# A decayed attention and two feed-forward layers on one core: the seventh Strassen-type product ahead of the second, and a new order of loads and VectorE work in the attention

## The reference, cut to what matters

```
for each block of 64 rows:                        # 2 batches, 8 heads, 768 rows, width 64
    intra = ((q k^T) * Dmask) v                   # Dmask[i,j] = lam^(i-j) for i >= j
    inter = (q * lam^(pos+1)) state
    out   = intra + inter
    state = lam^64 * state + (k * lam^(63-pos))^T v
x = out as [1536, 512]
p = probs / (sum(probs) + 1e-9)
x = sum over 4 experts e of  p[:, e] * (relu(x @ w1[e]) @ w2[e])     # w1 512x1024, w2 1024x512
h = x @ w_in;  out = (h * cos(h)) @ w_out                           # 512x2048, 2048x512
```

## Time and profile before

| | us |
|---|---|
| median of 3 runs | 815.4 (815.35 to 815.62) |
| the profiled execution | 815.58 |
| its span, first to last instruction | 813.8 |
| PE busy in it | 802.8 |
| attention, to the first matmul of the expert layer | 0 to 48.88 |
| steps 0 and 1 of the expert layer | 48.88 to 78.64 |

### The profile page before, as it was taken

One profiled execution on the slowest core, in us unless ns is written; L12 is line 12 of the kernel. 1 busy time (PEld: TensorE's weight loads), 2 busy tenths in 40 slices (PEclk: granted clock), 3 DMA queues, 4 the chain that ended last, 5 costly groups with the idle time before them and its releaser, 6 DMA issues.

```text
span 813.8 us, 11375 instructions
## 1 busy us (share of the span) xinstructions
PE 802.8 (99%) x4404; PEld 677.9 (83%) x4404; DVE 584.4 (72%) x964; ACT 292.0 (36%) x548; POOL 225.7 (28%) x228
## 2 busy tenths in 40 slices
PE   8989999999999999999999999999999999999998
PEld 7878888888888888888888888888888888888886
DVE  6988767767667657657667667677777777777766
ACT  4743222322322322322322222246545454555442
POOL 4955433433433433433433433242000000000000
PEclk9999999999999999999999999999999999999999
DMA  9941211111101121011111011001011011100004
GB/s 325 334 136 40 65 28 39 39 66 39 40 27 39 27 78 39 27 39 40 27 39 39 26 40 39 27 27 26 27 39 39 27 27 39 38 27 27 1 0 155
DMA packets 19865, 44.83 MB, mean 55 GB/s; under 512 B 2344, under 2 KB 2392, under 8 KB 19812
## 3 DMA queue, kind: packets, MB, share of 16 engines
q1 hardware_dynamic: 19812, 44.10, 17.0%
HBM read 40.93 MB, written 3.17 MB: 54 GB/s over the span
## 4 chain that ended last, share of the span: by engine, by line
PE 96%; DMA 2%; DVE 1%; POOL 0%; issue 0%; ACT 0%; SPq 0%; DVEq 0%
PE ps L982 32%; PE ps L963 28%; PE ps L1043 16%; PE ps L1062 16%; DMA att<-att_in 2%; PE ps L880 1%; PE ps L930 1%; PE ps L904 1%; PE ps L917 1%; PE ps L894 1%; DVE w_lo L673 0%; DVE temps L729 0%; POOL h_lo L422 0%; DVE att L633 0%; DVE temps L724 0%
## 5 line engine op out<-in xcount | busy, mean ns | idle before, releaser
L422 POOL TENSOR_TENSOR h_lo<-temps,h_hi 128x512 fp32r<-128x512 f32 (+1 forms) x128 | 135.1, 1056 | 298.7 <-ACT h_hi L518 298.7
L518 ACT ACTIVATE h_hi<-temps 128x512 fp32r<-128x512 f32 (+1 forms) x128 | 67.3, 525 | 338.9 <-DVE temps L729 338.9
L712 DVE TENSOR_TENSOR y<-ps,y 128x512 f32<-128x512 f32 x180 | 124.1, 689 | 71.7 <-PE ps L982 71.7
L963 PE MATMUL ps<-x_hi,w_hi 128*128 128x512 f32 (+1 forms) x448 | 150.4, 336 | 2.5 <-DVE temps L762 2.2
L982 PE MATMUL ps<-h_hi,w_hi 128*128 128x512 f32 x384 | 150.5, 392 | 0.8 <-POOL h_lo L422 0.8
L963 PE MATMUL ps<-x_hi,w_lo 128*128 128x512 f32 (+1 forms) x448 | 150.5, 336 | 0.0
L963 PE MATMUL ps<-x_lo,w_hi 128*128 128x512 f32 (+1 forms) x448 | 150.5, 336 | 0.0
L982 PE MATMUL ps<-h_lo,w_hi 128*128 128x512 f32 x384 | 150.4, 392 | 0.0
L982 PE MATMUL ps<-h_hi,w_lo 128*128 128x512 f32 x384 | 149.4, 389 | 0.0
L963 PEld LDWEIGHTS ps<-x_hi,w_hi 128*128 128x128 f32 x448 | 84.7, 189 | 15.2 <-DVE temps L762 2.6
L963 PEld LDWEIGHTS ps<-x_lo,w_hi 128*128 128x128 f32 x448 | 84.7, 189 | 11.7
(11 more groups left out here) (83 smaller groups left out, 1115.9 us busy)
## 6 DMA issues: line engine op xcount, KB each, us to landing
w_raw<-w_in SPq DMA_DIRECT2D x96, 256.0 KB, 2.6
att<-att_in SPq DMA_DIRECT2D x24, 512.0 KB, 6.4
temps<-p_scr SPq DMA_DIRECT2D x4, 768.0 KB, 4.0
out<-y SPq DMA_DIRECT2D x12, 256.0 KB, 2.0
att<-dp_in SPq DMA_DIRECT2D x1, 24.0 KB
p_scr<-att SPq DMA_DIRECT2D x1, 24.0 KB
lam<-lam_in SPq DMA_DIRECT2D x1, 6.0 KB, 1.8
```

Source lines behind the costliest of these rows:

```text
L422: pool.tensor_tensor(hs_lo[side][:, f, at], ring(s, i), f32(hs_hi[side][:, f, at]), ALU.subtract).then_inc(s_hlo, 1)
L518: act.activation(hs_hi[s % SIDES][:, f, at], ring(s, i), ACT.Copy).then_inc(s_hhi, 1)
L712: dve.tensor_tensor(at, from_bank, at, ALU.add).then_inc(s_y, 1)
L963: mm = pe.matmul(ps[:, bank, 0:CTS[side]], ww[q % 2][:, of], xx[side][:, 2 * x + k, :], start=(opens and k == 0 and n == 0), stop=(k == 1 ...
```

## The change

- The product order is P1, P6, P5, P7, P2, P4, P3 in all 32 steps. In side 0, down 0 now follows P5 and down 1 follows P7, and none follows P2; in side 1, down 0 follows P5, down 1 P7, downs 2 and 3 P2. Step 1 has its own list (`FOLLOW_FIRST`): 0 and 1 after P2, 2 to 4 after P4, 5 to 7 after P3. DVE's order follows: v2, v3, sum_of 1, a down piece, weighted 0.
- The first weights of the second product (w2 of quarter 0) are split during the attention: high parts by ACT and low parts by POOL in block 4, where DVE made the low parts in step 0.
- `qk(0)` is loaded in two halves of 256 KB; `scores(0)` starts on the first. After `kv(0)` come now `qk(2)`, `kv(1)`, `dps` (before: `dps`, `kv(1)`, `qk(2)`).
- DVE: the four scans for `qpow` are put around mask(1); in each block `k_decay(2p+3)` goes behind both masks; `x_parts` becomes `x_sums` (four sums) and `x_lows` (two low parts); the last piece of the first w1 weights goes between x_sums(4) and x_lows(4); x_lows(5) goes behind v2 of step 0. ACT does t_high(4) before x_high(5).
- PE's wait for the low parts of the x combinations (`s_tlo`) moves from P1 to P6.

```diff
-P1, P6, P5, P2, P7, P4, P3 = range(7)
+P1, P6, P5, P7, P2, P4, P3 = range(7)
-FOLLOW = (((), (), (), (0,), (1,), (2,), (3,)), ((), (), (0,), (1,), (2, 3), (4, 5), (6, 7)))
+FOLLOW = (((), (), (0,), (1,), (), (2,), (3,)), ((), (), (0,), (1,), (2, 3), (4, 5), (6, 7)))
+FOLLOW_FIRST = ((), (), (), (), (0, 1), (2, 3, 4), (5, 6, 7))
...
+            def load_qk0(half, signal):
+                at = slice(D // 2 * half, D // 2 * (half + 1))
+                sp.dma_start(qk[:, 0, :, at], att_in[0, :, 0:2, at]).then_inc(signal, 16)
...
-            load_qk(0)
+            load_qk0(0, s_qk_half)
+            load_qk0(1, s_qk[0])
             load_qk(1)
             load_kv(0)
+            load_qk(2)
+            load_kv(1)
             sp.dma_start(dps, dp_in).then_inc(s_dp, 16)
-            load_kv(1)
-            load_qk(2)
...
+            def w2_low(i):
+                hi, lo, raw = w2_split(0, i)
+                pool.wait_ge(s_whi, w2_count(0, i))
+                pool.wait_ge(s_wlo, w1_count(0) + i)
+                pool.tensor_tensor(lo, raw, f32(hi), ALU.subtract).then_inc(s_wlo, 1)
...
+                if p == BLOCKS - 2:
+                    w2_low(0)
+                    w2_low(1)
...
+                if p:
+                    t_high(p - 1)
                 if 0 < p < BLOCKS - 1:
-                    t_high(p - 1)
                     new_state(p)
                 x_high(p)
...
+                if p == BLOCKS - 2:
+                    w2_piece(0, 0)
+                    w2_piece(0, 1)
...
             for p in range(1, BLOCKS):
-                x_parts(p - 1)
+                x_sums(p - 1)
+                if p == BLOCKS - 1:
+                    w1_piece(0, 2)
+                x_lows(p - 1)
+                if p + 1 < BLOCKS:
+                    mask(2 * p + 2)
+                    if p == 1:
+                        dve.wait_ge(s_norm, 1)
+                        dve.reciprocal(dsum[:, :], dsum[:, :]).then_inc(s_norm, 1)
+                    if 2 <= p <= 3:
+                        w1_piece(0, p - 2)
+                    mask(2 * p + 3)
                 if p + 2 < BLOCKS:
                     k_decay(2 * p + 3)
...
-                dve.wait_ge(s_prod, 7 * s + P2 + 1)
+                dve.wait_ge(s_prod, 7 * s + P7 + 1)
+                dve.tensor_tensor(v3, bank_b, p1, ALU.add).then_inc(s_u, 1)
...
+                sum_of(s, 1, bank_c, v3)
+                if s == 1:
+                    down(0, 0)
                 if side == 1:
                     down(s - 1, 1)
                 else:
                     down(s - 1, 0)
-                dve.wait_ge(s_prod, 7 * s + P7 + 1)
-                dve.tensor_tensor(v3, bank_b, p1, ALU.add).then_inc(s_u, 1)
-                dve.wait_ge(s_u, 2 * s + 2)
-                sum_of(s, 1, bank_c, v3)
+                dve.wait_ge(s_prod, 7 * s + P2 + 1)
+                weighted(s, 0, bank_a)
...
-                    if i == P5 and side == 1:
+                    if i == (P2 if s == 1 else P5) and side == 1:
                         pe.wait_ge(s_wlo, w2_count(q, 1))
```

More of the change, by code:

```diff
@@ L37 @@
 STEPS = SIDES * QUARTERS
-P1, P6, P5, P2, P7, P4, P3 = range(7)
-PRODUCTS = ((0, 0, 0, True), (4, 4, 1, True), (3, 3, 2, True), (1, 1, 0, False), (5, 5, 1, False),
+P1, P6, P5, P7, P2, P4, P3 = range(7)
+PRODUCTS = ((0, 0, 0, True), (4, 4, 1, True), (3, 3, 2, True), (5, 5, 1, False), (1, 1, 0, False),
             (2, 6, 1, False), (6, 2, 2, False))
-FOLLOW = (((), (), (), (0,), (1,), (2,), (3,)), ((), (), (0,), (1,), (2, 3), (4, 5), (6, 7)))
+FOLLOW = (((), (), (0,), (1,), (), (2,), (3,)), ((), (), (0,), (1,), (2, 3), (4, 5), (6, 7)))
+FOLLOW_FIRST = ((), (), (), (), (0, 1), (2, 3, 4), (5, 6, 7))
 DOWNS = (8, 4)
@@ L154, in build @@
         s_qk = [sem(f"s_qk{i}") for i in range(QK)]
+        s_qk_half = sem("s_qk_half")
         s_kv = [sem(f"s_kv{i}") for i in range(KV)]
@@ L530, in _ @@
                 if s == 0:
-                    t_high(BLOCKS - 2)
                     t_high(BLOCKS - 1)
-                    w2_piece(0, 0)
                     h_high(s, 0)
-                    w2_piece(0, 1)
                     h_high(s, 1)
@@ L645, in k_decay, with x_sums @@
                                   ALU.mult).then_inc(s_kd[1], 1)
-            def x_parts(p):
-                side, at = x_columns(2 * p)
+            def x_sums(p):
                 b0, b1 = x_of(2 * p), x_of(2 * p + 1)
@@ L657, in x_parts, with x_lows @@
                 dve.tensor_tensor(t2, b1[:, 1, :, :], t1, ALU.subtract).then_inc(s_tsum, 1)
+                dve.wait_ge(s_tsum, 4 * p + 3)
+                dve.tensor_tensor(t4, b0[:, 1, :, :], t2, ALU.subtract).then_inc(s_tsum, 1)
+            def x_lows(p):
+                side, at = x_columns(2 * p)
+                b0, b1 = x_of(2 * p), x_of(2 * p + 1)
                 dve.tensor_tensor(tiles(xs_lo[side][:, 0:4, at]), b0, f32(tiles(xs_hi[side][:, 0:4, at])),
                                   ALU.subtract).then_inc(s_xlo, 1)
-                dve.wait_ge(s_tsum, 4 * p + 3)
-                dve.tensor_tensor(t4, b0[:, 1, :, :], t2, ALU.subtract).then_inc(s_tsum, 1)
                 dve.tensor_tensor(xs_lo[side][:, 4:6, at], b1[:, 1, :, :], f32(xs_hi[side][:, 4:6, at]),
@@ L673, in w2_piece, with q_powers @@
                 dve.tensor_tensor(lo, raw, f32(hi), ALU.subtract).then_inc(s_wlo, 1)
[L675 to L678, removed]
+            def q_powers(a):
                 dve.tensor_tensor_scan(qpow[:, a, :], lam[:, HEADS + a:HEADS + a + 1].to_broadcast([P, P]),
                                        zeros, 1.0, ALU.mult, ALU.add).then_inc(s_tab, 1)
+            mask(0)
+            q_powers(0)
+            q_powers(1)
+            mask(1)
+            q_powers(2)
+            q_powers(3)
+            k_decay(1)
             mask(2)
             mask(3)
-            dve.wait_ge(s_norm, 1)
-            dve.reciprocal(dsum[:, :], dsum[:, :]).then_inc(s_norm, 1)
             k_decay(3)
             for p in range(1, BLOCKS):
-                x_parts(p - 1)
+                x_sums(p - 1)
[10 more added lines that the diff above has]
+                    mask(2 * p + 3)
                 if p + 2 < BLOCKS:
                     k_decay(2 * p + 3)
[L690 to L698, removed]
+            x_sums(BLOCKS - 1)
             def down(s, i):
@@ L741, in _ @@
                 dve.tensor_tensor(v2, bank_b, p1, ALU.add).then_inc(s_u, 1)
+                if s == 0:
+                    x_lows(BLOCKS - 1)
                 if s == 1:
@@ L748, in _ @@
                     w2_piece(q + 1, 0)
-                if side == 1:
+                if side == 1 and s > 1:
                     down(s - 1, 0)
-                dve.wait_ge(s_prod, 7 * s + P2 + 1)
+                dve.wait_ge(s_prod, 7 * s + P7 + 1)
+                dve.tensor_tensor(v3, bank_b, p1, ALU.add).then_inc(s_u, 1)
                 if 4 * s >= R_RING:
                     dve.wait_ge(s_hlo, 4 * s - R_RING + 1)
-                weighted(s, 0, bank_a)
-                if s == 0:
-                    w2_piece(0, 0)
+                dve.wait_ge(s_u, 2 * s + 2)
+                sum_of(s, 1, bank_c, v3)
+                if s == 1:
+                    down(0, 0)
                 if side == 1:
@@ L872, in scores @@
                 s = n % QK
-                pe.wait_ge(s_qk[s], 16 * (n // QK + 1))
-                if n >= 1:
+                if n == 0:
+                    pe.wait_ge(s_qk_half, 16)
+                else:
+                    pe.wait_ge(s_qk[s], 16 * (n // QK + 1))
                     pe.wait_ge(s_mask, 2 * n - 1)
                 for a in range(PAIRS):
+                    if n == 0 and a == PAIRS // 2:
+                        pe.wait_ge(s_qk[0], 16)
                     for par in range(2):
@@ L996, in _ @@
                             pe.wait_ge(s_xlo, 2 * sum(SIDE_BLOCKS[:side + 1]))
-                            pe.wait_ge(s_tlo, sum(SIDE_BLOCKS[:side + 1]))
                         if s >= 1:
@@ L1001, in _ @@
                         pe.wait_ge(s_wlo, w1_count(0))
+                    if i == P6 and q == 0:
+                        pe.wait_ge(s_tlo, sum(SIDE_BLOCKS[:side + 1]))
                     if i == P6 and s >= 1:
                         pe.wait_ge(s_t, 3 * s - 1)
-                    if i == P5 and side == 1:
+                    if i == (P2 if s == 1 else P5) and side == 1:
                         pe.wait_ge(s_wlo, w2_count(q, 1))
@@ L1017, in _ @@
                     product(s, i)
-                    for d in FOLLOW[side][i]:
+                    for d in (FOLLOW_FIRST if s == 1 else FOLLOW[side])[i]:
                         down(s - 1, d)
```

## The result

The changed kernel takes 828.6 us (median of 4 runs, 826.6 to 829.6) against 815.4 us before (815.1 to 815.6): ratio 1.0159, 95% interval 1.0139 to 1.0179. It is slower, as forecast, but by 13.2 us where 6.7 were forecast, and above the end of the range at 825.0. The profiled execution took 826.59 us, with a span of 824.8 us. Its span is 11.0 us longer than that of before.

What follows compares the result with a forecast made beforehand. PE, busy 99% of the span, was taken as the bound. Attention -0.65, steps 0 and 1 -1.95 and steady steps +9.3 summed to +6.7 us, 822.1 us; own range 818.5 to 825, 8-in-10 range 812.3 to 825.

Steps and rivals of the forecast that it cites:

- The steady steps: Steps 2 to 31: each of 15 side-1 steps loses 0.62 us (bounds 0 and 0.9), +9.3 us in all.
- Steps 1 to 3 of its chain: Steady steps: DVE's row just fits, h_low 0 moves to 306.66 into w1 piece 1, and DVE and POOL take turns.
- step 4: Steady steps, turns applied: w1 piece 1 ends at 308.55, weighted 2 at 310.25, weighted 3 at 313.1 instead of about 312.17.
- The sign that I had named: Changed profile's list of PE waits: P7 waits for v2 about 15 times, 0.3 to 0.9 us each.
- the opening step: Whole kernel: PE is busy 99% of the span, so any new wait of PE is lost one for one.
- rival (c): Attention and steps 0 and 1: late w2 low parts and late dps eat both gains; 824.7 us, chance 0.07.
- The mask: Attention: mask(4) no longer stands behind k_decay(5), so scores(5) follows from_scores(3) at once; -1.09 us, bounds 0 and 1.1.
- The dps term: Attention: dps lands about 11.4 instead of 8.89, delaying the q_decays and scores(4); +0.45 us, bounds 0 and +0.8.
- Steps 0 and 1: First two expert steps: P4's 2.18 us wait goes, P7 of step 1 is next; -1.95 us, between -1.2 and -2.8.
- (a): Rival: w1 piece 1 slips in before h_low 0, no steady loss; 812.8 us, 811.5 to 814.2, chance 0.25.
- (b): Rival: waits of 0.1 to 0.25 us in 15 steps cancel the start's gain; 814.3 to 817 us, chance 0.13.
- The rows at 79 us: Kernel before's trace: POOL's sum ran between two queued DVE weight pieces, taken to show a second DVE instruction doesn't exclude POOL.

Runs made afterwards that it cites:

- masks_only: The kernel before with one edit, the key decay behind both masks in each attention block: 814.53 us, ratio 0.9988.
- dps_back: The changed kernel with the old product order from step 2 on and the dps load right behind kv(0) again: 813.56 us, ratio 0.9976.
- after_again: The changed kernel run once more, unedited, for its median: 827.38 us (4 runs), ratio 1.0145.
- prod1_first: The changed kernel with ACT taking prod1 of the side-1 step before h_high 3 of the step before: 822.43 us (1 run).
- low01_cleared: The changed kernel with h_low 0 and 1 of side-0 steps from 2 on replaced by memsets: 814.57 us (1 run).
- both_fixes: The changed kernel with w1 piece 1 right behind piece 0 and prod1 taken before h_high 3: 816.88 us (11 runs), 1.0019 of before.
- low0_cleared: The changed kernel with only h_low 0 of side-0 steps from 2 on replaced by a memset: 824.98 us (1 run).
- new_on_before: The kernel before with the new product order and DVE's new order in steps 2 to 31 alone: 827.81 us, ratio 1.0148.
- piece1_early: The changed kernel with w1 piece 1 made right behind piece 0, out of POOL's way: 823.67 us (1 run).

## Why the prediction was wrong in size

**The steady steps: right mechanism, the term was mis-sized.** "The side-1 step loses 0.62 us" measured 0.83. Steps 1 to 3 of its chain held within 0.01 us: h_low 0 starts at 306.65 in the prediction's times (306.66 forecast) and w1 piece 1 ends at 308.55, as forecast. Then step 4 failed by its own adding up. sum 2 starts at 308.47, as forecast, and at 0.60 us apiece weighted 2 starts at 309.67 and ends 0.68 later at 310.35, where I wrote 310.25; the trace has 310.35 (218.59 + 0.68). sum 3 then ends at 312.09 and weighted 3 at 313.29, where I wrote 313.1. That makes 0.19 us, most of the missing 0.21, with no new behaviour behind it; the rest is small change between the end of v2 and the start of P7. The 0.1 for a restarted PE was right (0.11). The sign that I had named, 15 waits of 0.3 to 0.9 us, came as 15 waits of 0.19 us on average, and the opening step, that a wait of PE is lost one for one, was wrong: idle time of 5.3 us stands against a loss of 12.5. 15 x 0.21 = 3.2 us, half of what the whole forecast lacks.

**The range.** The upper bounds of the three terms were +13.5 (0.9 per step), 0 and -1.2; their sum, +12.3, ends at 827.7. I closed the range at 825.0, with rival (c), and so left the bound of the largest term out. Even 827.7 is 0.9 below the median.

**The start: one half right, one half too cheap.** The mask was worth what was forecast: from scores(4) to scores(5) are 4.14 us in after (18.78 to 22.92) against 5.30 before, and masks_only alone gave -1.1 us. The dps term was +0.45 forecast. The timeline of after, POOL:

```profile
12.11 0.76 POOL L375 TENSOR_TENSOR dsum<-att 12x128 f32<-12x128 f32 x1 [10.64 <-DMA att<-dp_in]
...
14.61 2.50 POOL L363 TENSOR_TENSOR att<-att 128x512 f32<-128x512 f32 x2
```

and PE:

```profile
17.16 0.67 PE L927 MATMUL ps<-att 64*64 64x128 f32 x16 [0.57 <-POOL att L363]
...
18.78 1.16 PE L913 MATMUL ps<-att 64*128 64x128 f32 x16
...
26.43 1.16 PE L913 MATMUL ps<-att 64*128 64x128 f32 x16 [0.29 <-DMA att<-att_in]
```

dps landed at 12.1, not 11.4, and everything behind it followed as computed: scores(4) at 18.78 (18.15 forecast, 17.70 before), +1.08. That is past the bound that I had named for a slipped landing (+0.8): it slipped by 0.7 us, not by a third. Then came a cost that I had not seen, since of the late q_decay I followed only PE's wait: SP waits for it too, because qk(5) goes into the buffer of qk(2). SP's issues in after:

```profile
9.23 0.51 SPq L294 DMA_DIRECT2D att<-att_in  x1
15.97 0.33 SPq L287 DMA_DIRECT2D att<-att_in  x1
16.39 0.38 SPq L294 DMA_DIRECT2D att<-att_in  x1
16.82 0.90 SPq L304 DMA_DIRECT2D w_raw<-w_in  x2
17.82 0.92 SPq L287 DMA_DIRECT2D att<-att_in  x1
```

qk(5) is issued at 15.97 (13.93 before), right behind the end of q_decay(2) at 15.88, and the queue behind it goes late: kv(5), two weight pieces, and qk(6) at 17.82 (16.90 before). qk(6) lands 8.57 us later, at 26.39, and scores(6) waits 0.29 us. 0.63 and 0.29 turn -0.65 into about +0.3, which is the measured +0.30. dps_back gives about 1 us back: its q_decay(2) starts at 11.50, and it issues qk(5) at 12.86.

**Steps 0 and 1: right.** -1.79 measured, -1.95 forecast, with the collisions where they were put: the timeline of DVE in after, 57 to 62 us, has weighted 1 (L758) stretched by POOL's last t_low, which ends at 57.83, and weighted 2 and 3 by its h_lows. They end 0.5 to 0.6 us later than forecast, 0.3 of it from the later start. P7 of step 1 then waits 1.51 us for v2:

```profile
57.12 1.27 DVE L758 SCALAR_TENSOR_TENSOR temps<-temps 128x512 f32<-128x512 f32 x1
...
59.02 1.07 DVE L758 SCALAR_TENSOR_TENSOR temps<-temps 128x512 f32<-128x512 f32 x1
...
60.73 1.06 DVE L758 SCALAR_TENSOR_TENSOR temps<-temps 128x512 f32<-128x512 f32 x1
```

**The sum.** Forecast +6.7; the profiled execution has +0.3 - 1.8 + 12.5 = +11.0. The terms miss by 1.0, 0.2 and 3.2. The median lies 2.0 us above the profiled execution, while after_again's lies 0.5 above its own. The three slower runs of the first four (828.2 to 829.6 us) have a mean granted clock of 0.997 to 0.998; the fastest and all four of after_again (826.6 to 827.5) have 1.000. A mean of 0.998 over 825 us is one stretch of 3.3 us at half clock, an estimate, and such a stretch cost prod1_first 1.56 us (last section). That fits most of the 2.0, but these three runs have no trace, so it is not shown. Of the rivals, (a) and (b) are refuted by the 15 waits; (c) is refuted as a whole, since steps 0 and 1 kept their gain, but its half about the late dps was true.

**The rule of the Trainium skill.** That a VectorE instruction with two SBUF inputs and a GpSimd instruction that reads SBUF exclude each other was what gave the forecast its sign (the Trainium skill, "SBUF — State Buffer", "Who interferes with whom"). The traces agree: 0.42 to 1.53 us, and back to 0.41 in low01_cleared. The rows at 79 us, two DVE instructions in a row and POOL between them, carried over to the side-0 steps, where h_low 0 gets in ahead of w1 piece 1. They are no law, though: in the attention of both_fixes a DVE instruction lost its turn (below).

## What to carry to other kernels

Before moving a matmul forward, follow its operand back through the in-order queues: here P7's v2 hung on prod1, which stood behind h_high 3 on ACT, and P2 and down 1 had hidden that. A row of DVE work that just fits has no room for a single collision with POOL, and taking away one collision may only hand the time to the next; count a wait from start to start of PE's work, not by the idle time that the list shows: the list had 5.3 of 12.5 us, and none of the last 0.12 per quarter. A small load on which a queue of POOL work waits should not be put behind large ones, above all where later loads wait for that work to free their buffers.

## What the hardware showed that was not expected

- A POOL memset, which reads no SBUF, beside DVE work with two SBUF inputs costs the DVE work nothing: it runs beside a weighted of 0.68 and a weight piece of 0.42, and it takes 0.52 to 0.53 us itself in all 45 cases of low0_cleared and low01_cleared.
- DVE and POOL do not always take turns. In both_fixes, `k_decay(5)` (L667) waited while two POOL instructions ran one after the other, and took 2.90 us where it took 1.44 in after:

```profile
25.60 2.90 DVE L667 TENSOR_TENSOR att<-att,kpow 128x512 f32<-128x512 f32 x1
...
25.46 1.26 POOL L384 TENSOR_TENSOR att<-att,dsum 12x512 f32<-12x512 f32 x1
26.69 1.26 POOL L363 TENSOR_TENSOR att<-att 128x512 f32<-128x512 f32 x1
```

  prod1_first shows the same (2.66 us). In masks_only and low0_cleared the same pair met the same DVE instruction without a pause either, and DVE got its turn between them (1.81 and 1.43 us). In after a pause of 0.24 us lay between the two, since the second one's load landed late, and DVE went first. What decides the turn is open.
- After a pause of PE its granted clock was 0.5 (1.2 GHz) for about 3.4 us in some executions. The windows of prod1_first, where PE had paused 1.51 us until 64.25:

```profile
61.00:64.00 3.00, 1.62 (x12) 1.21 (x10) 2.00 (x4) 1.79 (x4) 3.00 (x3) 1.00 0.00 0
64.00:68.00 4.00, 3.75 (x15) 3.47 (x16) 3.26 (x5) 0.56 (x2) 3.92 (x5) 0.57 0.02 4
68.00:72.00 4.00, 4.00 (x22) 3.38 (x21) 1.71 (x3) 0.42 (x1) 0.84 (x2) 1.00 0.38 131
```

  Matmuls of 256 columns then start every 0.21 us instead of 0.12, and step 1 took 1.56 us longer. The same pause in the changed kernel (1.51 us until 63.23) was followed by full clock. new_on_before (59.5 to 62.9 us) and masks_only (58.0 to 61.4) had such a stretch behind their pause of 2.2 us, and before, with the same pause, had none. In those two the stretch cost nothing: steps 0 and 1 took 29.72 and 29.73 us with it, and 29.76 without it in before. piece1_early had one from 11.3 to 14.8 us, behind waits of 1.90 and 1.79 us for loads. What decides it is open.
- The same attention with the same order of loads took a different time from one execution to the next: with the changed kernel's attention the expert layer started between 49.18 and 50.8 us. Loads that landed at other times and the stretch at half clock account for piece1_early (50.8). both_fixes (50.3) and prod1_first (50.2) are late by the lost turn above: it held the masks behind k_decay(5), and PE waited 1.08 and 0.85 us for one of them ahead of scores(7).
